# Attention softmax kept in PSUM, and the woven attention units moved, in a fused attention and two-layer MLP kernel

## The reference

```python
def attention(q, k, v, mem_k, mem_v):          # B, H, S, D = 4, 8, 768, 64
    for c in range(S // 32):                   # chunks of 32 queries
        # keys: 8 memory keys and those from 16 left of the chunk to 8 right of it
        scores = (q_c @ k_full.T) / sqrt(D)
        a = exp(scores - max(scores))
        out_c = (a / (sum(a) + 1e-9)) @ v_full
x = attention(...)      # as [3072 tokens, 512]
h = x @ w_in                                   # 512 -> 2048
x = where(h > 0, h, exp(min(h, 0)) - 1) @ w_out
h = maximum(x @ w_in2, 0)
y = (s * h * h + b) @ w_out2
```

## Time and profile before

| | us |
|---|---|
| median of 3 runs | 1250.53 (1248.46 to 1257.01) |
| the profiled execution's own time | 1251.16 |
| its span in the profile | 1249.4 |
| mean granted TensorE clock, share of full speed | 0.958 |

### The profile page before, as it was taken

How to read it: one execution, slowest core, us unless ns; L and a number is a source line. 1 busy time by engine, 2 the same in 40 slices (tenths; PEclk the granted TensorE clock), 3 DMA queues, 4 the chain that set the end, 5 groups by cost and what they waited for, 6 DMA issues and landing times.

```text
span 1249.4 us, 17991 instructions
## 1 busy us (share of the span) xinstructions
PE 1133.7 (91%) x5755; PEld 893.5 (72%) x5755; DVE 866.5 (69%) x1245; ACT 754.2 (60%) x1774; POOL 444.6 (36%) x458
## 2 busy tenths in 40 slices
PE   7979688997889899969999999899999999999998
PEld 4656466775667677757778777678788787888886
DVE  5988256745796874779594894875957739657386
ACT  4876366655656755754675765646656557466463
POOL 6889155764334555553444134531001001000000
PEclk8995888998989989989999999999999999999999
DMA  9998588897869979966989669976668666686664
GB/s 216 262 267 234 140 264 269 283 348 237 280 214 285 305 251 304 312 218 196 391 281 297 185 194 364 318 207 194 172 206 289 191 189 173 190 241 187 190 189 161
DMA packets 203750, 302.80 MB, mean 242 GB/s; under 512 B 112520, under 2 KB 120712, under 8 KB 203656
## 3 DMA queue, kind: packets, MB, share of 16 engines
q1 hardware_dynamic: 203656, 301.65, 79.2%
HBM read 226.10 MB, written 75.50 MB: 241 GB/s over the span
## 4 chain that ended last, share of the span: by engine, by line
PE 46%; DVE 7%; DMA 4%; issue 3%; ACT 1%; POOL 0%; ACTq 0%; SPq 0%; DVEq 0%
PE ps L991 24%; PE ps L976 20%; DMA w_ring<-w_scratch 3%; DVE g_lo L1415 2%; DVE T L1410 1%; DVE X L1327 1%; PE ps L942 1%; DVE X L1410 1%; DVE xc_lo L1320 1%; DMA elu<-x_scratch 1%; ACT att L1065 0%; DVE y L1327 0%; DVE X L1384 0%; DVE X L1390 0%; ACT g_hi L1183 0%
## 5 line engine op out<-in xcount | busy, mean ns | idle before, releaser
L976 PE MATMUL ps<-xc_hi,w_ring 128*128 128x512 f32 x1344 | 442.6, 401 | 21.9 <-ACT s L1119 7.4
L991 PE MATMUL ps<-g_hi,w_ring 128*128 128x512 f32 x1344 | 430.7, 402 | 34.2 <-DVE g_lo L1415 19.1
L991 PEld LDWEIGHTS ps<-g_hi,w_ring 128*128 128x128 f32 x1344 | 252.6, 192 | 104.2 <-issue 36.5
L976 PEld LDWEIGHTS ps<-xc_hi,w_ring 128*128 128x128 f32 x1344 | 256.8, 191 | 83.7 <-issue 18.4
L991 PE MATMUL ps<-g_lo,w_ring 128*128 128x512 f32 x672 | 266.7, 397 | 0.0
L976 PE MATMUL ps<-xc_lo,w_ring 128*128 128x512 f32 x672 | 265.2, 395 | 0.0
L1415 DVE TENSOR_TENSOR g_lo<-X,g_hi 128x512 fp32r<-128x512 f32 x240 | 181.8, 763 | 57.6 <-ACT g_hi L1183 56.9
L763 POOL TENSOR_TENSOR w_new<-w_raw,w_new 128x256 fp32r<-128x256 f32 x170 | 154.4, 911 | 173.5 <-ACT w_new L1196 169.8
L1183 ACT ACTIVATE g_hi<-X 128x512 fp32r<-128x512 f32 x240 | 149.2, 627 | 76.1 <-PE ps L991 73.1
L1327 DVE TENSOR_TENSOR X<-s,ps 128x512 f32<-128x512 f32 x144 | 96.0, 681 | 103.8 <-ACT s L1125 77.4
L991 PEld LDWEIGHTS ps<-g_lo,w_ring 128*128 128x128 f32 x672 | 129.0, 192 | 28.3
(11 more groups left out here) (113 smaller groups left out, 1436.1 us busy)
## 6 DMA issues: line engine op xcount, KB each, us to landing
w_ring<-w_scratch SPq DMA_DIRECT2D x336, 512.0 KB, 4.1
w_scratch<-w_new SPq DMA_DIRECT2D x170, 256.0 KB, 5.0
w_scratch<-att SPq DMA_DIRECT2D x54, 256.0 KB, 4.8
w_raw<-in_moe_w_in SPq DMA_DIRECT2D x16, 512.0 KB, 5.7
w_raw<-in_moe_w_out SPq DMA_DIRECT2D x16, 512.0 KB, 5.8
x_scratch<-y SPq DMA_DIRECT2D x3, 2048.0 KB, 8.6
att<-x_scratch SPq DMA_DIRECT2D x6, 1024.0 KB, 8.4
out<-elu SPq DMA_DIRECT2D x24, 256.0 KB, 4.4
```

The costliest lines, as they stand in the source:

```text
L976: last = nc.tensor.matmul(bank_of(st.pi, st.i), w[:, a, cols], x[:, st.pi, kk, :], start=(st.pi in (P1, P5, P4) and kk == 0 and n == 0), s ...
L991: last = nc.tensor.matmul(bank_of(st.pi, d), w[:, a, cols], x[:, k % RING, :], start=(st.pi in (P1, P5, P4) and st.i == 0 and n == 0), sto ...
```

## The change

- Exponentials are written back into the score banks in PSUM. `normalise` reads them there and writes P to SBUF. `score(n)` in the head waits for `P_ready` of unit n-2 where it waited for `exp_done`; `exps` waits for the sums of unit n-2 where it waited for its P transposes; `normalise` takes that wait over. The 1e-9 stands in a second column beside the row sum, and a reduce over the two makes the total.
- Three idle products in each head iteration from 2 on, after the score, into bank 4 (behind the copy of the even P^T of unit it-2).
- 46 weight products are saved in the head, two and three an iteration by turns; 49 are prepared by GpSimd alone. P2 is prepared third. The saves of x0 of units 18 and 19, and the loads of unit 20, come one or two loads of weights later.
- Woven units begin at 10 + 14c for all twelve; the score and all that follows stand one step later.

```diff
-PREPARED = (P1, P4, P5, P6, P2, P7, P3)
+PREPARED = (P1, P4, P2, P5, P6, P7, P3)
...
-WOVEN = [(HEAD + c, 10 + 13 * c) for c in range(6)] + [(HEAD + 6 + c, PER_TILE + 2 + 14 * c) for c in range(6)]
-K_T, Q_T, SC, MAX, EXP_E, EXP_O, NORM, P_T, PV = 0, 1, 2, 3, 4, 5, 6, 9, 11
+WOVEN = [(HEAD + c, 10 + 14 * c) for c in range(12)]
+K_T, Q_T, SC, MAX, EXP_E, EXP_O, NORM, P_T, PV = 0, 1, 3, 4, 5, 6, 7, 10, 12
...
-HEAD_SAVES = 36
-HEAD_PREP = 42
+HEAD_SAVES = 46
+HEAD_PREP = 49
...
-        rowsum = sb("rowsum", [QU, 2, H])
+        rowsum = sb("rowsum", [QU, 2, H, 2])
+        total = sb("total", [QU, 2, H])
...
-                for _ in range(2):
+                for _ in range(2 + (it % 2)):
                     if saves < HEAD_SAVES:
...
-            for n in range(HEAD - 2, HEAD):
-                save_x0(n)
-
             for d in range(W_RING, STEPS // 2):
                 load_weights(d)
                 t, s = divmod(2 * d - 6, PER_TILE)
+                if W_RING < d <= W_RING + 2:
+                    save_x0(HEAD - 3 + d - W_RING)
                 for n, w0 in WOVEN:
-                    if n == HEAD and d == W_RING or n > HEAD and d == (WOVEN[n - HEAD - 1][1] + 10) // 2:
+                    if n == HEAD and d == W_RING + 1 or n > HEAD and d == (WOVEN[n - HEAD - 1][1] + 10) // 2:
                         load_qk(n)
-                    if n == HEAD and d == W_RING or n > HEAD and d == (WOVEN[n - HEAD - 1][1] + PV + 8) // 2:
+                    if n == HEAD and d == W_RING + 2 or n > HEAD and d == (WOVEN[n - HEAD - 1][1] + PV + 8) // 2:
                         load_v(n)
...
-                for pi in (P5, P6, P2):
+                for pi in (P2, P5, P6):
...
             def score(n):
                 if n < HEAD and n >= 2:
-                    pe.wait_ge(exp_done, n - 1)
+                    pe.wait_ge(P_ready, n - 1)
...
                     score(it + 1)
+                if 2 <= it:
+                    pe.wait_ge(PT_sb[0], it - 1)
+                    idle_products(3, bank[4])
...
-                    pe.wait_ge(exp_done, HEAD - 1)
+                    pe.wait_ge(P_ready, HEAD - 1)
                     step(0)
...
-            pe.wait_ge(exp_done, HEAD)
+            pe.wait_ge(P_ready, HEAD)
             step(2)
...
                     if n >= 2:
-                        act.wait_ge(PT_done[1], n + 1 - lag_of(n))
+                        act.wait_ge(sum_done, n + 1 - lag_of(n))
                 for h in range(PAIRS * e, PAIRS * e + PAIRS):
-                    last = nc.scalar.activation(P[i][:, h, :], S_of(n)[:, h, :], ACT.Exp, bias=nbias[:, i, h:h + 1],
-                                                accum_out=rowsum[:, i, h:h + 1])
+                    last = nc.scalar.activation(S_of(n)[:, h, :], S_of(n)[:, h, :], ACT.Exp, bias=nbias[:, i, h:h + 1],
+                                                accum_out=rowsum[:, i, h, 0:1])
...
-                nc.vector.tensor_scalar_add(rowsum[:, i, :], rowsum[:, i, :], 1e-9).then_inc(sum_done, 1)
+                nc.vector.tensor_reduce(out=total[:, i, :], in_=rowsum[:, i, :, :], axis=mybir.AxisListType.X, op=ALU.add)\
+                    .then_inc(sum_done, 1)
                 dve.wait_ge(sum_done, n + 1)
-                nc.vector.reciprocal(rinv[:, i, :], rowsum[:, i, :]).then_inc(rinv_done, 1)
+                nc.vector.reciprocal(rinv[:, i, :], total[:, i, :]).then_inc(rinv_done, 1)
                 dve.wait_ge(rinv_done, n + 1)
-                nc.vector.tensor_tensor(P[i], P[i], rinv[:, i, :].unsqueeze(2).to_broadcast([QU, H, KEYS]),
+                if n >= 2:
+                    dve.wait_ge(PT_done[1], n + 1 - lag_of(n))
+                nc.vector.tensor_tensor(P[i], S_of(n), rinv[:, i, :].unsqueeze(2).to_broadcast([QU, H, KEYS]),
                                         ALU.mult).then_inc(P_ready, 1)
```

More of the change, by code:

```diff
@@ L402, in build @@
         nat_zeros = sem("nat_zeros")
+        tiny_set = sem("tiny_set")
         qT_done = sem("qT_done")
@@ L1423, in _ @@
                 nc.vector.memset(v_of(n)[0:LEFT, :], 0.0).then_inc(pads, 1)
+            nc.vector.memset(rowsum[:, :, :, 1:2], 1e-9).then_inc(tiny_set, 1)
             dve.wait_ge(nat_zeros, 1)
+            dve.wait_ge(tiny_set, 1)
             for it in range(-2, HEAD + 1):
```

## The result

The changed kernel takes 1217.47 us (median; 1216.72 to 1219.03), the kernel before 1253.77 us in the same runs: a ratio of 0.972 (95% interval 0.967 to 0.976). The predicted 1242 us was a change of 9 us; measured were 36. The time lies at the lower end of the range, and the stages say which part of the forecast failed.

What follows compares the result with a forecast made beforehand. TensorE, busy 91%, was taken as the bound overall, with VectorE the engine to look at in the head. Head +18 us and tiles -27 (-5 -2 -6 +2 -5 -11) gave -9: 1251.2 to 1242 us, range 1216 to 1268.

Steps and rivals of the forecast that it cites:

- The score therefore leaves the shadow and joins the chain: Head: the score, waiting for the normalise of unit n-2, lengthens the cycle from 4.60 to 5.53 us.
- The 9 us for lower clock: Head: three of nine units' worth at 1.2 GHz, +9 us of the head's +18.
- With no unit in the last 24 steps VectorE should lag less: -5: Tiles, around step 206: TensorE's 8.1 us wait behind tile 2's x load should shrink, -5 us (0 to -8).
- unit 26 moves ...: +2: Tiles: unit 26 moves to steps 94 to 106, among tile 1's x splits, costing +2 us (0 to +5).
- P2 ahead of P5 and P6: -2 (0 to -6): Weights: ScalarE cuts one product that needs no sum while GpSimd makes the sums, -2 us (0 to -6).
- Waits of TensorE on it were 9.0 us ... -6: Woven units: scores two steps behind q's transposes give ScalarE's copy 1.37 us more, -6 us (0 to -9).
- The distances ... are unchanged, so the 9.5 us in front of the P transposes stay: Woven units: distances from score to exponential, transposes and P times V unchanged, so 9.5 us of waits remain.
- Clock in the tiles -11 (-3 to -18): Tiles: 22 us of 1.2 GHz stretches go with the gaps before them, -11 us (-3 to -18).
- The step-8 stall: First tile stage: stall about 2.5 us, since the first weight cut still waits for x0 of unit 19; -5 (0 to -7).
- The low clock from unit 9 on: Rival, chance 0.20: all nine head units from 9 on run at 1.2 GHz; head +35, tiles -20, 1266 us.
- The clock's holding: Rival, chance 0.20: no fall of the clock in the head; head +9, tiles -32, 1228 us.
- The waits only move: Rival, chance 0.20: ScalarE's in-order queue delays copies, waits reappear elsewhere; head +18, tiles -15, 1254 us.

Runs made afterwards that it cites:

- e12_wait_only: Kernel before with one line changed: head scores wait for the normalise of unit n-2, exponentials stay in SBUF; 1280.4 us, ratio 1.020.
- e4_no_idle: Changed kernel without the idle products; 1212.2 us, ratio 0.965.
- e17_p2_only: Kernel before with only P2 prepared third; 1235.2 us, ratio 0.983.
- e18_saves_only: Kernel before with 46 saves in the head, 49 products by GpSimd alone, later x0 saves and unit 20 loads, P2 in its old place; 1250.2 us, ratio 0.996.
- e7_offsets: Kernel before with woven units' score and all that follows one step later, old starts; 1256.8 us, ratio 1.002.
- e1_units: Kernel before with only the woven units' change: starts at 10 + 14c, score and what follows one step later; 1223.4 us, ratio 0.974.
- e5_both: Kernel before with the weights and woven-unit changes, without exponentials in PSUM or idle products; 1216.0 us, ratio 0.970.
- e6_starts: Kernel before with the twelve woven unit starts 14 steps apart, old offsets inside the unit; 1241.3 us, ratio 0.991.
- e13_phase16: e1_units with all unit starts six steps later, at 16 + 14c; 1242.0 us, ratio 0.989 to the kernel before.
- e10_late_wait: e4_no_idle with ScalarE's wait for the x0 save moved from the first weight cut to the fifth; 1207.6 us, ratio 0.963.
- e15_hidden_late: Changed kernel with idle products ahead of the score and the x0 wait moved to the fifth weight cut; 1201.7 us, ratio 0.957.
- e3_sbuf: Changed kernel with exponentials back in SBUF, the old score wait and the old addition of 1e-9; 1215.3 us, ratio 0.968.
- e11_sbuf_late: Changed kernel with exponentials in SBUF, total by a reduce, no idle products, x0 wait at the fifth weight cut; 1212.4 us, ratio 0.965.
- e9_idle_hidden: Changed kernel with the three idle products moved ahead of the score; 1205.6 us, ratio 0.960.

## Why the prediction was right and wrong

**The head was right by its own steps.** "The score therefore leaves the shadow and joins the chain": the masks are released by the normalise, the cycle is 5.63 us for 5.53, step 0 stands at 148.1 for 147, the low clock in the head stayed at about 40 us, and e12_wait_only shows the wait by itself (0.7 us a cycle at full clock). Idle products "all of it in the chain" for 0.70: 0.59 a cycle by e4_no_idle. The 9 us for lower clock can't be separated; the sum of the head was right with them.

**The normalise at a flat 1.22 us was right** (1220 to 1222 in 32 executions). The surcharge of about 0.065 us that I had worked out from the Trainium skill (VectorE: DVE Perf Modes, the TRN2 errata) did not appear: the trace disagrees, and the measurement decides. The stretching that went is what the Trainium skill (SBUF — State Buffer, "Who interferes with whom") describes, in my words: an instruction of VectorE with two SBUF inputs contends with GpSimd's reads, one with at most one SBUF input does not (outside the 2-port modes). The trace agrees: with one large SBUF input less, 1475 ns in the head's mean became 1220.

**"With no unit in the last 24 steps VectorE should lag less: -5", and "unit 26 moves ...: +2", left out the largest piece of part 4.** The stage from step 168 lost 12.4 us, because units' own products left a stage in which TensorE had hardly any idle time (52.2 us, busy 47.56), and the stage that took unit 26, priced at +2, got 1.7 us shorter, because TensorE had 8.6 us to spare there. The sum had no term for the first. The -5 itself, for the last stage, was about right (52.4 to 47.7).

**"P2 ahead of P5 and P6: -2 (0 to -6)" failed.** e17_p2_only measured -17 us in the tiles and -20 in all. The term was sized by the sums that ScalarE waits for. Those waits (10.2 us) did go, but the stages show at most 6 us where they stood; 9 us came in steps 112 to 224, and of the 17 in all 9.6 are busy time, that is, clock. Why a reorder of GpSimd's products shortens those steps stays open.

**"Waits of TensorE on it were 9.0 us ... -6" was right in size (9.0 to 2.4) and not in what it is worth.** I gave the whole wait to the distance of score and qT's transposes. The longest of the six, 3.63 us, stood behind a weight cut, and is gone in e17_p2_only and e18_saves_only with the old distance; e7_offsets, with the new distance alone, has 0.6 of the 9.0 left and gains nothing. The name in the releaser's column is the last instruction of a queue, not its cause.

**"The distances ... are unchanged, so the 9.5 us in front of the P transposes stay" failed.** They fell (6.7 to 0.7 on the P transposes, 9.9 to 2.4 on P times V in steps 0 to 224). It takes both parts: with part 4 alone (e1_units) the P transposes still wait 10.3 us, with e5_both 4.8. Distances in steps say how much time a unit's work has; how long it takes hangs on what else the engines do in those steps. e6_starts (-12), e7_offsets (+3), both (-32), and e13_phase16 (21 us slower than e1_units in these steps) show that part 4 is one edit, not the sum that I made: -6, +2, -5.

**"Clock in the tiles -11 (-3 to -18)" failed** in its size: low clock fell from 61.2 to 17.0 us, 20 us of TensorE's busy time. I had let it follow the waits, and half the waits were missing from the sum.

**The step-8 stall** was forecast at 2.5 us and is 5.3. The step was "about 4.5 of issues and landing" for the x0 save; ScalarE's wait for it is this, in the changed kernel:

```profile
ACT w_new L1200 <- DMA x_scratch<-att: 9.7, 1, 9.7
```

The mechanism (x0's landing takes the slot's place) was right, e10_late_wait shows it, and its size was short by 3 us.

**The signs and the rivals.** Of the signs for "right", all came but one: step 8 waits 5.3 us, not under 4. The low clock from unit 9 on did not come (0.83 in the second half of the normalises' stretch). The clock's holding did not come either in the head (0.86); in e15_hidden_late it nearly did (0.95). "The waits only move" is real for one edit, e7_offsets, and false for the whole.

**What stays open.** A shorter head gives part of its gain back in the tiles: e3_sbuf, e4_no_idle and e11_sbuf_late each start step 0 earlier by 12 to 18 us than the changed kernel and take 6.5 to 7.7 us more for steps 0 to 224. In e10_late_wait, which is e4_no_idle without the x0 wait at the first cut, it is 1.2, so for this pair the x0 save explains it. But e9_idle_hidden has that wait (4.5 us in front of step 8, for 6.4) and gives back only 2.4, and e11_sbuf_late doesn't have it and gives back 7.7. The traces show one thing in which the kernels with parts 3 and 4 and exponentials in SBUF (e3_sbuf, e5_both, e11_sbuf_late) differ from the changed kernel and e10_late_wait: in steps 0 to 224 ScalarE waits 5.6 to 6.3 us in three places for another of GpSimd's sums (0.4 in one), and the woven normalise takes 1456 to 1490 ns in the mean (1220). So part 1 may pay in the tiles what it costs in the head, by keeping VectorE and GpSimd out of each other's way; no run tests it. Why P2's place shortens steps 112 to 224 is open too. Why the start at step 10 suits and 16 doesn't was read from the waits, on X and g_lo, and not tested step by step.

## What to carry to other kernels

Compare the changed kernel with the old one stage by stage before pricing waits: side work costs its own products where TensorE is full, and little where it idles, so first ask in which stage it stands. An instruction in an in-order engine that waits for a slow helper delays whatever stands behind it: follow the idle time of the releaser's own engine before pricing a wait, and then check in the stage that the time came back. Starts and offsets of periodic work have to be judged together, on the chip, since each can uncover the wait that the other removes. Put filler products where TensorE waits anyway, never behind the instruction that ends the wait, and put a wait at the first use of the buffer that it protects.

## What the runs showed of the hardware that was not expected

Exponentials written to PSUM are a little shorter than those to SBUF. The row of the page, changed kernel, then before (count, busy us, mean ns, idle):

```profile
L1069 ACT ACTIVATE ps<-ps,nbias 96x128 f32<-96x128 f32 x256 | 85.3, 334 | 0.8 <-DVE nbias L1290 0.8
```

```profile
L1065 ACT ACTIVATE att<-ps,nbias 96x128 f32<-96x128 f32 x256 | 89.1, 365 | 1.2 <-DVE nbias L1286 1.2
```

The mean fell by 31 ns, 8%, on an engine that the head doesn't wait for.

Three products of 512 columns a cycle, 0.81 us, raised the mean granted clock of whole executions from 0.967-0.973 to 0.976-0.983 behind the score and to 0.979-0.984 in TensorE's wait ahead of it (four executions each). Behind the score they cost more than they gave back (5.3 us slower in all), ahead of it they cost nothing (6.5 us faster).

Two operations of GpSimd that take some 0.73 us each alone took 6.23 us together at 209 us of the kernel before, as two took 8.51 in the earlier trace rows. VectorE ran ten instructions there without a break, most of them with two SBUF inputs.
